# A 32-byte buffer of constants widened to 128 bytes, which moves every on-chip tile behind it by 96 bytes

## The chip, the cores and the metric

The kernel runs on one core of a Trainium2 chip. The metric is device time in microseconds, from one execution of the whole program; the time of a kernel is the median of its runs.

## The reference

Windowed attention with a distance bias, then two feed-forward blocks, all in float32.

```python
batch, n_heads, seq, head_dim = (4, 8, 576, 64)     # q, k, v
scores = scale * np.matmul(q, k.transpose(0, 1, 3, 2))
mask = (rel >= 0) & (rel < 128)
scores = np.where(mask, scores + bias[None], -1000000000.0)
attn = np.exp(scores - max) / (sum + 1e-09)
x = attn @ v                                        # as (2304 tokens, 512)

h = np.maximum(x @ w_in1, 0.0);  x = h * h @ w_out1       # w_in (512, 2048), w_out (2048, 512)
h = x @ w_in2;                   out = (h * np.cos(h)) @ w_out2
```

## The kernel before

**Attention.** The 32 heads are done in 16 pairs. For each pair p TensorE makes the scores of 576 tokens in bands of 192 keys (lines 534 and 543), VectorE adds the bias and takes the row's minimum (line 1089), ScalarE takes the exponent (line 821), GpSimd divides by the row's sum (line 508), TensorE transposes the probabilities (line 589) and multiplies by v (line 631). The probabilities of a pair lie in one of three buffers, probs0 to probs2, taken in turn by p modulo 3. TensorE works on pair s's scores, pair s-2's transposes and pair s-3's values in one turn.

**The two blocks.** They run as 2 x 24 steps (`mlp_step`): three groups of 768 tokens, with eight steps each, per block. A step makes 2 x 128 hidden units. The product with w_in is one level of Strassen's scheme: seven products (`hidden_product`, line 693), each of six matmuls of 384 columns. Float32 is split into a high and a low part in the float32r format, and a product is hi x hi, hi x lo and lo x hi for each of two slices of 128 in the contraction. In the trace's names the moving operand stands first and the weights second: `psum<-xt_hi,comb` streams xt_hi over weights comb.

- The moving high part is always in `xt_hi0` or `xt_hi1` (by the group's parity).
- The moving low part is in `x_lo` for the products 0, 2, 4 and 6 of a step, and in `xt_lo0` or `xt_lo1` for the products 1, 3 and 5.
- The weights are always in `comb`.

After each product stand one to three pieces of the second product (`second_product`). In the first block a piece is three times a 512-column and a 256-column matmul that stream g_hi or g_lo over weights `wout` (lines 732 and 734). In the second block it is the other way round: three 512-column matmuls that stream `wout` over weights g_hi or g_lo (line 727). In a step with `n % STEPS == 1` the pieces stand otherwise: product 0 has three behind it there.

**Where the tiles lie.** `place` hands out addresses within a partition one behind the other, in the order in which it is called, and nothing but the sizes decides them:

```python
            if at is None:
                offset, top[0] = top[0], top[0] + size
```

In the built program `x` starts at byte 16512 = 129 x 128. x, x_lo, raw, sums, angle, the three kept_out tiles, comb, wout and ident lie ahead of `consts`, and all of them start at multiples of 128. `consts` starts at 111232 (also one) and has 32 bytes, of which columns 0 to 2 hold three constants that ScalarE reads as its bias (lines 898, 904, 914). All that is placed behind it starts past a multiple of 32.

The order of work on each of the five engines' queues is written out by hand, and instructions wait on semaphores by count.

Of the kernel before, what the change touches and what calls it, by code (L numbers as in the profile page):

```python
# [15 lines left out]
F32 = mybir.dt.float32  # L16
# [5 lines left out]
P = 128  # L22
# [89 lines left out]
def attention_mlp_kernel(nc, q_t, k_t, v, w_in1, w_out1, w_in2, w_out2, out):  # L112
    with ExitStack() as ctx:
# [3 lines left out]
        def place(name, shape, dtype, at=None):  # L117
            size = 4 * math.prod(shape[1:])
            if at is None:
                offset, top[0] = top[0], top[0] + size  # L120
            else:
                offset, at[0] = at[0], at[0] + size
            return nc.alloc_sbuf_tensor_at(name, shape, dtype, offset=offset)
# [16 lines left out]
        wout = place("wout", [P, W_RING, 2, DM], F32R)  # L140
        wout_raw = place("wout_raw", [P, W_RING, 2, DM], F32, wout_at)
        ident = place("ident", [P, P], F32)
        consts = place("consts", [P, 8], F32)
        part_a = place("part_a", [P, NH], F32)
        part_b = place("part_b", [P, NH], F32)
        xt_hi0 = place("xt_hi0", [P, 7, 2, NH], F32R)
# [1339 lines left out]
```

## Time and profile before

| | |
|---|---|
| runs | 868.67, 868.55, 868.83 us; median 868.67 us |
| profiled execution | 868.67 us, of which its span 866.6 us |
| TensorE busy with matmuls | 852.7 us, 98% of the span |
| weight loads (beside the matmuls) | 768.2 us |
| VectorE, ScalarE, GpSimd busy | 649.2, 525.7, 79.1 us |
| attention alone | about the first 91 us, then overlapped with the first step |

The span runs from the first to the last instruction; the device time is 2.1 us more. "Busy" of TensorE includes the depth of its pipeline: matmuls overlap, so the time that one takes of a stream is read from the start of one to the start of the next, not from its own duration.

### The profile page before, as it was taken

To read this page: it belongs to the slowest core of one execution; us is meant where nothing else is said; L and a number is where in the kernel's file an instruction comes from. 1 tells how busy PE (TensorE), PEld (TensorE's weight loads), DVE (VectorE), ACT (ScalarE), POOL (GpSimd) and SP (SyncE) were. 2 spreads that over 40 slices of the span, in tenths; PEclk is the share of its full clock that TensorE was granted. 3 is DMA by queue.
4 is the path that set the end of the run, shared out by engine and by line. 5 is a ranking of instruction groups with operands and counts; after the bars stand their busy time and mean duration, and the time that the engine had idled before them with its cause. 6 is when DMAs were issued, how large, how long until landed. Compare 5 with 4: busy or idle time off the path is not lost.

```text
span 866.6 us, 16159 instructions
## 1 busy us (share of the span) xinstructions
PE 852.7 (98%) x5844; PEld 768.2 (89%) x5844; DVE 649.2 (75%) x1455; ACT 525.7 (61%) x1145; POOL 79.1 (9%) x174
## 2 busy tenths in 40 slices
PE   7999999999999999999999999999999999999997
PEld 5888998999999999999999989988899898898996
DVE  6999878787677676786776777777877777767664
ACT  7999544342253433343333787777888777777774
POOL 6678600000000000000000000000000000000000
PEclk9999999999999999999999999999999999999999
DMA  6775825647588688688678555555566555664522
GB/s 226 229 250 168 292 84 195 227 166 245 202 291 290 235 305 303 218 290 314 234 254 305 193 181 180 185 196 184 188 236 195 172 178 189 219 230 167 194 73 73
DMA packets 72046, 185.34 MB, mean 214 GB/s; under 512 B 7200, under 2 KB 19488, under 8 KB 69920
## 3 DMA queue, kind: packets, MB, share of 16 engines
q1 hardware_dynamic: 71104, 183.23, 61.8%
q8 instruction: 47, 0.77, 0.4%
q10 hardware_dynamic: 864, 1.08, 0.3%
q14 instruction: 31, 0.25, 0.1%
HBM read 141.82 MB, written 42.47 MB: 213 GB/s over the span
## 4 chain that ended last, share of the span: by engine, by line
PE 89%; DVE 5%; ACT 2%; issue 2%; DMA 1%; DVEq 0%
PE psum L693 37%; PE psum L727 21%; PE psum L732 13%; PE psum L734 7%; PE psum L631 4%; PE psum L589 3%; PE psum L534 3%; DVE hidden_sum L1214 1%; DVE g_lo L1268 1%; DMA wout_raw<-w_out 1%; ACT probs L821 1%; PE psum L543 1%; DVE kept L1193 0%; DVE xt_raw L1133 0%; DMA k_raw<-k_t 0%
## 5 line engine op out<-in xcount | busy, mean ns | idle before, releaser
L693 PE MATMUL psum<-xt_hi,comb 128*128 128x384 f32 x1344 | 397.5, 337 | 3.9 <-DVE hidden_sum L1214 3.7
L693 PEld LDWEIGHTS psum<-xt_hi,comb 128*128 128x128 f32 x1344 | 247.4, 188 | 21.6 <-issue 7.9
L727 PE MATMUL psum<-wout,g_hi 128*128 128x512 f32 x576 | 180.2, 394 | 0.3 <-DVE g_lo L1268 0.3
L732 PE MATMUL psum<-g_hi,wout 128*128 128x512 f32 x384 | 149.8, 393 | 0.0
L1268 DVE TENSOR_TENSOR g_lo<-work,g_hi 128x384 fp32r<-128x384 f32 x192 | 102.5, 553 | 60.2 <-ACT g_hi L922 58.6
L922 ACT ACTIVATE g_hi<-work 128x384 fp32r<-128x384 f32 x192 | 97.0, 516 | 71.4 <-DVE work L1255 39.6
L693 PE MATMUL psum<-x_lo,comb 128*128 128x384 f32 x384 | 129.0, 336 | 0.0
L727 PEld LDWEIGHTS psum<-wout,g_hi 128*128 128x128 f32 x576 | 105.9, 188 | 12.4 <-issue 0.7
L727 PE MATMUL psum<-wout,g_lo 128*128 128x512 f32 x288 | 113.9, 395 | 0.0
L734 PE MATMUL psum<-g_hi,wout 128*128 128x256 f32 x384 | 107.9, 281 | 0.0
L693 PE MATMUL psum<-xt_lo,comb 128*128 128x384 f32 x288 | 96.9, 336 | 0.0
L834 ACT ACTIVATE part_a<-psum 128x384 f32<-128x384 f32 x48 | 23.5, 490 | 100.7 <-PE psum L693 100.6
L732 PEld LDWEIGHTS psum<-g_hi,wout 128*128 128x128 f32 x384 | 71.9, 187 | 9.7
L1214 DVE TENSOR_TENSOR part_b<-psum,part_a 128x384 f32<-128x384 f32 x48 | 26.8, 558 | 65.5 <-PE psum L693 65.5
L693 PEld LDWEIGHTS psum<-x_lo,comb 128*128 128x128 f32 x384 | 72.2, 188 | 3.8
L732 PE MATMUL psum<-g_lo,wout 128*128 128x512 f32 x192 | 75.3, 392 | 0.0
L734 PEld LDWEIGHTS psum<-g_hi,wout 128*128 128x128 f32 x384 | 72.2, 188 | 0.0
L909 ACT ACTIVATE angle<-angle 128x384 f32<-128x384 f32 x96 | 49.8, 519 | 34.9 <-DVE angle L1247 34.7
L508 POOL TENSOR_SCALAR probs<-probs,inverse 128x192 f32<-128x192 f32 (+1 forms) x144 | 67.7, 492 | 20.3 <-DVE inverse L1101 20.3
L727 PEld LDWEIGHTS psum<-wout,g_lo 128*128 128x128 f32 x288 | 54.1, 188 | 12.8
L821 ACT ACTIVATE probs<-probs,neg_max 128x192 f32<-128x192 f32 (+1 forms) x144 | 61.7, 431 | 5.6 <-DVE neg_max L1089 5.6
L914 ACT ACTIVATE angle<-angle,consts 128x384 f32<-128x384 f32 x96 | 59.1, 616 | 2.7
(96 smaller groups left out, 1280.5 us busy)
## 6 DMA issues: line engine op xcount, KB each, us to landing
comb<-comb SPq DMA_DIRECT2D x80, 768.0 KB, 5.0
wout<-wout SPq DMA_DIRECT2D x48, 512.0 KB, 4.9
comb<-comb SPq DMA_DIRECT2D x8, 1792.0 KB, 7.1
comb<-kept SPq DMA_DIRECT2D x8, 1792.0 KB, 6.9
wout_raw<-w_out SPq DMA_DIRECT2D x48, 256.0 KB, 6.2
comb<-comb SPq DMA_DIRECT2D x40, 256.0 KB, 3.1
v_raw<-v SPq DMA_DIRECT2D x16, 512.0 KB, 3.5
raw<-w_in SPq DMA_DIRECT2D x32, 256.0 KB, 7.2
```

The costliest lines, as they stand in the source:

```text
L508: pool.tensor_scalar(m, m, inverse[:, r, u:u + 1], 1.0, ALU.mult, ALU.mult).then_inc(probs_ready, 1)
L631: return pe.matmul(psum[D * h:D * h + D, O_BANK + n % 2, HALF * (n // 2):HALF * (n // 2) + HALF], block, m[block.base_partition():block.ba ...
L693: last = pe.matmul(psum[:, H_BANK + i % 2, 0:NH], wi, mi[:, k, :], start=first, stop=True, skip_group_check=True)
L727: last = pe.matmul(psum[:, Y_BANK + c, :], g[:, r, tok], w, start=start and m == 0, stop=True, skip_group_check=True)
L732: pe.matmul(psum[:, Y_BANK + c, :], wi[:, w], g[:, r, 0:512], start=start and m == 0, stop=True, skip_group_check=True)
L734: last = pe.matmul(psum[:, Y_BANK + 4 + c // 2, 256 * (c % 2):256 * (c % 2) + 256], wi[:, w], g[:, r, 512:N], start=start and m == 0 and c ...
L821: act.activation(m, m, ACT.Exp, bias=neg_max[:, r, u:u + 1], scale=-1.0, accum_out=row_sum[:, r, u:u + 1]).then_inc(exp_ready, 1)
L909: act.activation(a, a, ACT.Abs).then_inc(abs_ready, 1)
L914: act.activation(a, a, ACT.Sin, bias=consts[:, 0:1], scale=-1.0).then_inc(cos_ready, 1)
L922: act.activation(g_hi[:, r, cols], work[i][:], ACT.Copy).then_inc(g_hi_ready, 1)
L1214: dve.tensor_tensor(to, psum[:, H_BANK + bank, 0:NH], left, ALU.add).then_inc(sum_done, 1)
L1268: dve.tensor_tensor(g_lo[:, r, cols], work[i][:], g_hi[:, r, cols].bitcast(F32), ALU.subtract)\
```

## The change

```diff
         ident = place("ident", [P, P], F32)
-        consts = place("consts", [P, 8], F32)
+        consts = place("consts", [P, 32], F32)
         part_a = place("part_a", [P, NH], F32)
```

No instruction is added, removed or moved: the sequence on each of the five engines is the same, shapes and waits too. Only addresses differ, by 96 bytes, for all tiles placed behind `consts`. Where they start in the built programs, as what is left over a multiple of 128 bytes:

| tile | used for | before | after |
|---|---|---|---|
| x, x_lo, comb, wout, ident, raw, sums, angle, kept_out | see above | 0 | 0 (not moved) |
| part_a, part_b, part_c, hidden_sum, work | VectorE, ScalarE | 32 | 0 |
| xt_hi0, xt_hi1, xt_lo0, xt_lo1 | moving operands of line 693 | 32 | 0 |
| g_hi, g_lo | moving (732, 734), weights (727) | 32 | 0 |
| kept | source of a DMA | 32 | 0 |
| probs0, probs1, pt0, pt1, v_raw, v_first | attention | 32 | 0 |
| probs2, q_raw, k_raw, bias, bias_first, bias_tail | attention | 64 | 32 |

The last row is behind `slopes`, which has 32 bytes of its own: the operands of the scores are not at multiples of 128 after the change.

## Rows read from the trace of the kernel before

**Rows 1.** The page's head and its first part: busy time of TensorE.

```profile
span 866.6 us, 16159 instructions
PE 852.7 (98%) x5844; PEld 768.2 (89%) x5844; DVE 649.2 (75%) x1455; ACT 525.7 (61%) x1145; POOL 79.1 (9%) x174
```

**Rows 2.** Windows: busy us (count) of PE, PEld, DVE, ACT, POOL, clock, DMA.

```profile
290.00:490.00 200.00, 199.48 (x1142) 185.19 (x1141) 143.04 (x253) 80.60 (x144) 0.00 (x0) 0.95 0.76 269
520.00:840.00 320.00, 319.48 (x1584) 286.38 (x1583) 234.34 (x452) 245.67 (x464) 0.00 (x0) 0.95 0.56 187
```

**Rows 3.** The waits of PE: us in total, times, longest; its largest.

```profile
PE psum L693 <- DVE hidden_sum L1214: 3.7, 8, 1.1
```

**Rows 4.** Groups by form of PE: busy us, mean ns, idle before.

```profile
L732 PE MATMUL psum<-g_hi,wout 128*128 128x512 f32 x384 | 149.8, 393 | 0.0
L693 PE MATMUL psum<-x_lo,comb 128*128 128x384 f32 x384 | 129.0, 336 | 0.0
L727 PE MATMUL psum<-wout,g_lo 128*128 128x512 f32 x288 | 113.9, 395 | 0.0
L693 PE MATMUL psum<-xt_lo,comb 128*128 128x384 f32 x288 | 96.9, 336 | 0.0
```

**Rows 5.** Timeline of PE in the first block: start, us, what.

```profile
401.57 0.34 PE L693 MATMUL psum<-xt_hi,comb 128*128 128x384 f32 x1
401.75 0.33 PE L693 MATMUL psum<-xt_lo,comb 128*128 128x384 f32 x1
...
402.62 0.39 PE L732 MATMUL psum<-g_hi,wout 128*128 128x512 f32 x1
...
403.66 0.33 PE L693 MATMUL psum<-xt_hi,comb 128*128 128x384 f32 x1
403.83 0.33 PE L693 MATMUL psum<-x_lo,comb 128*128 128x384 f32 x1
...
404.70 0.39 PE L732 MATMUL psum<-g_hi,wout 128*128 128x512 f32 x1
```

**Rows 6.** Timeline of PE in the second block.

```profile
701.93 0.34 PE L693 MATMUL psum<-xt_hi,comb 128*128 128x384 f32 x1
702.12 0.34 PE L693 MATMUL psum<-xt_lo,comb 128*128 128x384 f32 x1
...
703.00 0.62 PE L727 MATMUL psum<-wout,g_hi 128*128 128x512 f32 x2
...
704.39 0.34 PE L693 MATMUL psum<-xt_hi,comb 128*128 128x384 f32 x1
704.57 0.34 PE L693 MATMUL psum<-x_lo,comb 128*128 128x384 f32 x1
...
705.44 0.63 PE L727 MATMUL psum<-wout,g_hi 128*128 128x512 f32 x2
```

**Rows 7.** Timeline of PE in the second block, a step with `n % STEPS == 1`.

```profile
741.45 0.34 PE L693 MATMUL psum<-xt_hi,comb 128*128 128x384 f32 x1
741.62 0.33 PE L693 MATMUL psum<-xt_lo,comb 128*128 128x384 f32 x1
...
742.49 0.62 PE L727 MATMUL psum<-wout,g_hi 128*128 128x512 f32 x2
```

**Rows 8.** Chain that ended last, in the attention: start, us, what.

```profile
64.72 1.04 PE psum L589 x8
...
70.34 1.04 PE psum L589 x8
...
75.96 1.04 PE psum L589 x8
```

**Rows 9.** Groups by form of DVE.

```profile
L1173 DVE TENSOR_TENSOR comb<-raw,comb 128x768 fp32r<-128x768 f32 x8 | 7.6, 953 | 0.0
L1193 DVE TENSOR_TENSOR kept<-raw,kept 128x768 fp32r<-128x768 f32 x8 | 7.6, 952 | 0.0
```

**Rows 10.** DMA issues: count, KB each, median us to landing.

```profile
comb<-comb SPq DMA_DIRECT2D x8, 1792.0 KB, 7.1
comb<-kept SPq DMA_DIRECT2D x8, 1792.0 KB, 6.9
```

## The prediction

> **What bounds the kernel now.** I read the page's first part before anything else, since it tells which engine has no slack: TensorE is busy for 852.7 of 866.6 us [rows 1]. Then the windows, for whether that holds in each stage: in 200 us of the first block it is busy for 199.48, in 320 us of the second for 319.48, while VectorE is busy for 143.04 and 234.34 and ScalarE for 80.60 and 245.67 [rows 2]. So both have over a fifth of each window free. The granted clock is 0.95 of the full 2.4 GHz level in both windows, so the level does not change. Then TensorE's waits: the largest is for VectorE's sums, 3.7 us in all [rows 3]. What decides the time is therefore how fast TensorE streams its operands, and nothing else. That is the one place in which an address could matter, and the rest of the reading is for that.
>
> Own durations are of little use there: they contain the pipeline's depth. I read starts in the timeline. A product of line 693 is six matmuls of 384 columns, and its time is from its first start to the start of what follows it.
>
> - First block: a product with xt_lo runs from 401.57 to 402.62, 1.05 us; the piece behind it, 3 x (512 + 256) columns, to 403.66, 1.04 us; a product with x_lo to 404.70, 1.04 us [rows 5].
> - Second block: a product with xt_lo from 701.93 to 703.00, 1.07 us; two pieces, 6 x 512 columns, to 704.39, 1.39 us; a product with x_lo to 705.44, 1.05 us [rows 6].
> - Second block, another order of pieces: a product with xt_lo from 741.45 to 742.49, 1.04 us [rows 7].
>
> **The change part by part.** No instruction is added or moved, so there is no term for work, and no queue is passed. What is left is the price of a start 32 bytes past a multiple of 128. The trace of before has tiles of both kinds in the same work, so it can be read.
>
> *Moving operands of the hidden products.* In a step 34 of 42 matmuls stream xt_hi or xt_lo, both at 32; the other 8 stream x_lo, at 0. Over 48 steps that is 1632 at 32 and 384 at 0, and the weights, comb, are at 0 for all. A product with x_lo has two matmuls at 0, one with xt_lo has none, and the rest of it is alike. If the start had a price, the products with xt_lo would always be longer by twice that price. They are longer by 0.01 us in the first block and by 0.02 in the second [rows 5, 6], which would make 5 and 10 ns per matmul. But the product with xt_lo at 741.45 takes 1.04 [rows 7], less than the one with x_lo at 704.39, minus 5 ns by the same division. And the same product with xt_lo, with every start the same, takes 1.05, 1.07 and 1.04 us in these three places. Thus where it stands in the sequence moves it by up to 0.03 us, more than the contrast between the tiles. Times are rounded to 0.01 us. The mean durations agree: 336 ns with x_lo and 336 with xt_lo [rows 4]. The two ends of the price are minus 5 and plus 10 ns; I take 0, since the sign changes with the place while the addresses stay.
>
> *The second products.* In the first block g is the moving operand (at 32) and wout the weights (at 0): 2304 columns in 1.04 us are 0.451 ns per column. In the second block wout is the moving operand (at 0) and g the weights (at 32): 3072 columns in 1.39 us are 0.453 ns per column [rows 5, 6]. The durations of 512 columns are 393 and 395 ns [rows 4]. The roles are exchanged and the rate isn't. This does not exclude that both roles cost the same, since one of the two is at 32 in either block; but in the product with x_lo two of six matmuls have both operands at 0, and it takes 1.04 us for 2304 columns, 0.451 ns per column, too. I take 0 for the 1152 matmuls of the first block and the 864 of the second.
>
> *Attention.* The transposes of three pairs in turn, whose probabilities lie in probs buffers at 32, 32 and 64, take 1.04 us for eight each time, and start 5.62 us apart [rows 8]. A weight operand's start at 32 or 64 is worth less than 10 ns in eight. q_raw and k_raw go from 64 to 32, v_raw and pt from 32 to 0; no aligned counterpart exists in the trace for them. Nearest are the hidden products above: 5 ns of 173 is 3%, and of a turn of 5.62 us over 16 pairs that is at most 2.7 us either way. I take 0 for this too, by the transposes.
>
> *VectorE and ScalarE.* The split of the weights takes 953 ns into comb (at 0) and 952 ns into kept (at 32) [rows 9]. Price 0, and it would be covered: VectorE has 57 of 200 us free in the first block [rows 2]. Without that cover, 1 ns on each of its 1455 instructions would be 1.5 us.
>
> *DMA.* Of the moved tiles kept is the large one: eight transfers of 1792 KB out of it take 6.9 us, and the same transfer out of comb, at 0, takes 7.1 [rows 10]. They are covered either way, since TensorE's largest wait is for VectorE [rows 3].
>
> The Trainium skill says otherwise of such a transfer (DMA: Bandwidth & Descriptors, "How a descriptor splits into AXI transactions"): a descriptor that starts off a multiple of 256 bytes fetches from the boundary below it, and the unused bytes cost beats. kept goes from 160 to 0 past such a multiple, so by the page its reads would become a little shorter. The trace has the unaligned one shorter by 0.2 us, so it does not show this; and with TensorE not waiting for it, the sum is the same by either.
>
> The sum: 868.67 + 0. The profiled execution took 868.67 us, 866.6 of span and 2.1 around it, which is also the median of the three runs, so nothing has to be corrected. I say 868.6.
>
> **The rivals.**
>
> *A, faster: the products' time does depend on the placement, in the block where it is longest.* For it: in the second block the products take 1.05 and 1.07, and 1.04 occurs with the same operands [rows 6, 7], so something costs up to 0.03 us there, and the longer ones are those with no moving operand at 0. Against it: the first block has the same starts and does without. If all went at 1.04: 72 products with xt_lo by 0.03 and 96 with x_lo by 0.01 are 2.2 + 1.0 = 3.1 us, to 865.6.
>
> *B, much faster: all that TensorE loses against its clock is the price of the starts.* At 0.95 x 2.4 = 2.28 GHz and one column per cycle six times 384 columns are 1.01 us, 2304 are 1.01 and 3072 are 1.35. Saved: 168 products of the first block by 0.035, 168 of the second by about 0.05, 192 pieces of 2304 columns by 0.03 and 144 times 3072 columns by 0.04, or 5.9 + 8.4 + 5.8 + 5.8 = 26 us, to 843. Against it: matmuls with both operands at 0 do not go faster than the others [rows 5].
> [...]
>
> *C, slower: the pattern of the second block gets into the first.* The place in the sequence decides between 1.04, 1.05 and 1.07, for a reason that the trace doesn't show. If that reason has to do with how the starts of two operands stand to each other, making all equal can put both blocks at the longer values: 72 x 0.02 + 96 x 0.01 = 2.4 us in the first block, to 871.1. It decides from the point where more than 0.005 us is added per product on average (336 x 0.005 = 1.7 us). The operands of the scores, 64 to 32, could add at most 2.7 us in the same direction. Against it: x_lo, comb and wout already start at multiples of 128 together, and their products are among the shortest.
>
> *D: the change doesn't do what it says.* It is so for attention: q_raw and k_raw start at 32 after it. For the blocks the starts do become multiples of 128. D gives 868.7 and can't be told from no effect.
>
> **How the numbers follow.** A measurement here can tell about 0.2% (1.7 us) from no change. No effect, D with it: 0.76, own range 867.1 to 870.3. A: 0.10, B: 0.02, C: 0.12. Half of A stays close enough to be out by more than 0.2% and above 866. So faster by over 0.2% has 0.12, within it 0.76, slower 0.12. The range is 866.0 to 871.0: it holds the first case whole, half of A and most of C, and leaves out B, the rest of A and the far end of C, under 2 in 10.
>
> **What would show it.** In the profile of the changed kernel the products should again be 1.04 to 1.07 us from start to start in the same places as before, 6 x 512 columns 1.39, a turn of the attention 5.62, and the windows 199.5 of 200 and 319.5 of 320. Under A products with xt_lo in the second block fall to 1.04; under B everything, to 1.01; under C products of the first block rise to 1.05 and 1.07. My prediction is wrong if line 693's starts move nearer or farther by more than 1 ns on average with the clock still at 0.95, or if TensorE gets a new wait of over 2 us.

## The result and the profile after

The changed kernel takes 870.79 us (median of 22 runs, 869.26 to 871.35), the kernel before 868.67 us on the same chip. The ratio is 1.0025, with a 95% interval from 1.0018 to 1.0031: slower by 2.1 us, a quarter of a per cent. The forecast was 868.6 us and no effect; 870.79 lies inside the range, but the direction is rival C's.

The page of the changed kernel, head and first part, as [rows 1] of before:

```profile
span 868.9 us, 16159 instructions
PE 853.8 (98%) x5844; PEld 770.1 (89%) x5844; DVE 649.1 (75%) x1455; ACT 525.4 (60%) x1145; POOL 79.3 (9%) x174
```

Nothing is done more often, VectorE and ScalarE are as busy as before, and TensorE still has no slack, as its windows say too (columns as in [rows 2]):

```profile
290.00:490.00 200.00, 199.54 (x1137) 185.35 (x1136) 143.38 (x255) 79.92 (x143) 0.00 (x0) 1.00 0.77 270
520.00:840.00 320.00, 319.57 (x1584) 286.28 (x1583) 234.22 (x453) 245.74 (x465) 0.00 (x0) 1.00 0.57 189
```

What differs in the first window is the count: about five matmuls fewer than in [rows 2] fit into the same 200 us. The granted clock is 1.00 where it was 0.95, and the kernel is slower all the same; more on that below. The timeline of TensorE in the first block, in the places of [rows 5]:

```profile
403.31 0.34 PE L693 MATMUL psum<-xt_hi,comb 128*128 128x384 f32 x1
403.48 0.34 PE L693 MATMUL psum<-xt_lo,comb 128*128 128x384 f32 x1
...
404.36 0.39 PE L732 MATMUL psum<-g_hi,wout 128*128 128x512 f32 x1
...
405.41 0.34 PE L693 MATMUL psum<-xt_hi,comb 128*128 128x384 f32 x1
405.59 0.34 PE L693 MATMUL psum<-x_lo,comb 128*128 128x384 f32 x1
...
406.46 0.40 PE L732 MATMUL psum<-g_hi,wout 128*128 128x512 f32 x1
```

A product is 1.05 us with xt_lo as with x_lo, and the piece between them 1.05. Two decimals are too coarse here. From the starts to the nanosecond, the median over the steps 3 to 23 is 1.039 us before and 1.046 after for a product with x_lo, 1.042 and 1.053 for one with xt_lo. These values are nearly constant: the same from step to step to 1 or 2 ns, outside of the steps with `n % STEPS == 1` and of 13 of the 147 products, which take some 0.08 us more in both kernels. In the second block, in the places of [rows 6]:

```profile
704.20 0.34 PE L693 MATMUL psum<-xt_hi,comb 128*128 128x384 f32 x1
704.37 0.34 PE L693 MATMUL psum<-xt_lo,comb 128*128 128x384 f32 x1
...
705.25 0.62 PE L727 MATMUL psum<-wout,g_hi 128*128 128x512 f32 x2
```

This one is 1.05 us (1.052 in the median) where it was 1.07 (1.062), while the products with x_lo went from 1.049 to 1.054: the second block changed too, but the changes nearly cancel. (Medians of the second block, here and below, are over the steps 26 to 33. With x_lo that before is one of two values: the products 2 and 4 of a step take 1.046 us, 0 and 6 take 1.049.) In the place of [rows 7], the other order of pieces, the product is longer than before, 1.06 for 1.04:

```profile
743.71 0.34 PE L693 MATMUL psum<-xt_hi,comb 128*128 128x384 f32 x1
743.88 0.34 PE L693 MATMUL psum<-xt_lo,comb 128*128 128x384 f32 x1
...
744.77 0.40 PE L727 MATMUL psum<-wout,g_hi 128*128 128x512 f32 x1
```

Where the 2.1 us are is read best from the starts of whole steps, here step 3, step 24 (the first of the second block) and step 46 of the changed kernel:

```profile
138.52 0.41 PE L693 MATMUL psum<-xt_hi,comb 128*128 128x384 f32 x1 [1.18 <-DVE hidden_sum L1214]
...
471.65 0.34 PE L693 MATMUL psum<-xt_hi,comb 128*128 128x384 f32 x1
...
819.48 0.34 PE L693 MATMUL psum<-xt_hi,comb 128*128 128x384 f32 x1
```

and of the kernel before, in the second profile that was taken of it (below):

```profile
138.23 0.41 PE L693 MATMUL psum<-xt_hi,comb 128*128 128x384 f32 x1 [1.12 <-DVE hidden_sum L1214]
...
469.86 0.33 PE L693 MATMUL psum<-xt_hi,comb 128*128 128x384 f32 x1
...
817.34 0.34 PE L693 MATMUL psum<-xt_hi,comb 128*128 128x384 f32 x1
```

A step of the first block went from (469.86 - 138.23) / 21 = 15.792 to (471.65 - 138.52) / 21 = 15.863 us, one of the second from (817.34 - 469.86) / 22 = 15.795 to 15.810. Over 24 steps each that is 1.7 + 0.4 = 2.1 us, the whole loss. Of the longer step of the first block, 66 ns are in its seven hidden products and 6 ns in the pieces between them; in the second block it is 9 and 6 ns. In what follows "step 1" and "step 2" are these two numbers.

### The profile page after: what moved, and what is told of

Its sections match the earlier page's. It is cut to its first block, busy times and chain, and to the rows that moved or that the text cites. A ratio compares the mean times of both kernels' runs of the same rounds, so it can differ in the third digit from the quotient of the medians.

```text
span 868.9 us, 16159 instructions
## 1 busy us (share of the span) xinstructions
PE 853.8 (98%) x5844; PEld 770.1 (89%) x5844; DVE 649.1 (75%) x1455; ACT 525.4 (60%) x1145; POOL 79.3 (9%) x174
## 4 chain that ended last, share of the span: by engine, by line
PE 87%; DVE 7%; issue 2%; ACT 2%; DMA 1%; POOL 0%; DVEq 0%
PE psum L693 37%; PE psum L727 21%; PE psum L732 13%; PE psum L734 7%; PE psum L631 4%; PE psum L589 3%; PE psum L534 2%; DVE hidden_sum L1214 1%; DVE g_lo L1268 1%; DMA wout_raw<-w_out 1%; DVE probs L1089 1%; DVE xt_raw L1133 0%; DVE kept L1193 0%; PE psum L543 0%; DMA k_raw<-k_t 0%
```

## The experiments

### Four other widths of the same buffer

If a start's place over a multiple of 128 bytes were what counts, a shift by 128 would change nothing, and 224 would be as good as 96.

```diff
-        consts = place("consts", [P, 8], F32)
+        consts = place("consts", [P, 16], F32)   # w16; 24, 40 and 64 in w24, w40 and w64
```

> consts is 64 bytes wide, so all that lies behind it is moved by 32 bytes and starts at 64 over a multiple of 128. Theory 1 (the start over a multiple of 128 bytes sets the few ns between matmuls): something between the kernel before and the changed one or of its own, a product of the first block between 1.040 and 1.062 us from start to start, and a turn of the attention between 5.55 and 5.62. Theory 2 (it is the position modulo a longer period or against the tiles that don't move): can't be told apart by this run alone. Rival 3 (the difference is not of the addresses but of how single executions fall out): 868.7, products 1.040 and 1.042 in the first block as before.

> consts is 96 bytes wide, moved by 64 bytes, start at 96 over a multiple of 128. Theory 1: a time of its own, within 2.5 us of the kernel before; the products of the first block a fixed value in all steps. Theory 2: the same. Rival 3: 868.7 and the product times of before.

> consts is 160 bytes wide, moved by 128 bytes: every tile starts at the same place over a multiple of 128 as in the kernel before, but not over a multiple of 256. Theory 1: as before, 868.7 us (within 0.5), products of the first block 1.040 and 1.042 us, a turn of the attention 5.62. Theory 2: differs from before in the product times by 3 ns or more. Rival 3: as before too.

> consts is 256 bytes wide, moved by 224 bytes, all tiles of the blocks start at multiples of 128 as in the changed kernel, but 128 bytes farther. Theory 1: as the changed kernel, 870.8 us (within 0.5), products of the first block 1.046 and 1.053 us, a turn of the attention 5.55. Theory 2: product times of its own. Rival 3: 868.7.

| kernel | shift, bytes | median us | ratio to before (95%) | step 1 | step 2 |
|---|---|---|---|---|---|
| before | 0 | 868.29 | | 15.792 | 15.795 |
| w16 | 32 | 869.51 | 1.0012 (0.9999 to 1.0026) | 15.854 | 15.802 |
| w24 | 64 | 872.75 | 1.0051 (1.0034 to 1.0068) | 15.929 | 15.853 |
| changed kernel | 96 | 870.79 | 1.0025 (1.0018 to 1.0031) | 15.863 | 15.810 |
| w40 | 128 | 867.97 | 1.0003 (0.9994 to 1.0013) | 15.823 | 15.784 |
| w64 | 224 | 866.58 | 0.9978 (0.9966 to 0.9989) | 15.754 | 15.755 |

The changed kernel's own runs of before had 868.67. Theory 1 falls twice. With 224 bytes the blocks' tiles start at multiples of 128 as in the changed kernel, and the time is 4 us less, also less than that of before. And with 128 bytes the total is that of before by accident: a product with x_lo in the first block takes 1.055 us, not 1.039, one with xt_lo in the second 1.046, not 1.062. The effect of a placement is real and of both signs: 6 us lie between w24 and w64. w24 is 4.5 us above before, outside of the 2.5 us that its expectation gave.

### What has a period, and what counts: shifts of 256 and 512, and a shift of everything

```diff
+        consts = place("consts", [P, 72], F32)    # w72: all behind it by 256 bytes; 136 in w136: by 512
```
```diff
+        front = place("front", [P, 24], F32)      # front96: x and all behind it by 96 bytes, consts as before
         x_at = [top[0]]
```

> The kernel before, unchanged, profiled once more. The profile that was shown of it has a granted clock of 0.95 throughout, and a turn of the attention of 5.62 us where four kernels with other addresses have 5.55. If the turn follows the addresses it is 5.62 again; if it belongs to that one execution it is 5.55, with the products of the blocks at 1.039, 1.042, 1.049 and 1.062 us again if these follow the addresses.

> consts is 288 bytes wide, the tiles behind it are moved by 256 bytes. Theory 2a (the period is 256 bytes): product times of the kernel before to 1 ns, and its time within 0.5 us. Theory 2b (the distance to the tiles that don't move matters, without a period of 256): product times of its own. Theory 1 (period 128) was against the run with 128 bytes already and would give those of before here too.

> consts is 544 bytes wide, moved by 512 bytes. If there is a period of 512 bytes: the product times of the kernel before to 1 ns and its time within 0.5 us. If there is none: times of its own, between 864.5 and 873 us as the widths so far.

> consts stays at 32 bytes, and a pad of 96 bytes stands ahead of x, so that every tile, x, comb and wout included, is moved by 96 bytes: the starts of xt and g over a multiple of 128 are those of the changed kernel (0), those of x, comb and wout become 96, and all distances between tiles are those of the kernel before. If distances between tiles that TensorE reads together decide: the product times of the kernel before (1.039, 1.042, 1.049, 1.062) and 868.3 us. If each tile's own start decides: different from both, by 3 ns or more in a product.

| kernel | median us | ratio (95%) | step 1 | step 2 | product times, ns: x_lo, xt_lo; second block x_lo, xt_lo |
|---|---|---|---|---|---|
| before_again | 868.73 (1 run) | | 15.792 | 15.795 | 1039, 1042; 1049, 1062 |
| w72 | 868.06 | 0.9999 (0.9990 to 1.0008) | 15.795 | 15.795 | 1039, 1042; 1049, 1062 |
| w136 | 867.91 | 0.9997 (0.9987 to 1.0007) | 15.791 | 15.795 | 1039, 1042; 1049, 1062 |
| front96 | 867.77 | 1.0000 (0.9990 to 1.0009) | 15.795 | 15.795 | 1039, 1042; 1049, 1062 |

The runs of before beside these three had 868.04 us. All four kernels have the same product times to the nanosecond. The timeline of w72 shows two of them, 401.72 to 402.76 with xt_lo and the next from 403.81:

```profile
401.72 0.34 PE L693 MATMUL psum<-xt_hi,comb 128*128 128x384 f32 x1
401.90 0.33 PE L693 MATMUL psum<-xt_lo,comb 128*128 128x384 f32 x1
...
402.76 0.39 PE L732 MATMUL psum<-g_hi,wout 128*128 128x512 f32 x1
...
403.81 0.33 PE L693 MATMUL psum<-xt_hi,comb 128*128 128x384 f32 x1
```

So at the kernel's own distance the address acts modulo 256 bytes, and it is no single start: in front96 xt and g start at the same place over a multiple of 128 as in the changed kernel, and nothing is lost, because x, comb and wout moved with them. What counts is how the tiles stand to each other. The table of starts modulo 128 hides that: modulo 256, x_lo, comb and wout start at 128 in both kernels, and xt and g go from 160 to 0. I call distance the start of xt or g minus that of comb or wout, modulo 256. It is 32 before (160 against 128), 64 in w16, 96 in w24, 128 in the changed kernel, 160 in w40 and 0 in w64. In the pieces of the second block wout is the moving operand and g the weights, so there the moving operand stands at minus this distance.

before_again was for a second matter. The profile that the prediction was made from has a granted clock of 0.95, here it is 1.00, and the turn of the attention is 5.55 us (60.88 to 66.43 in the chain):

```profile
60.88 2.16 PE psum L631 x64
...
66.43 2.16 PE psum L631 x64
```

It was 5.62 there, and is 5.55 in the median in all 17 other traces of a whole kernel. So the turn belongs to that one execution, and not to addresses, while the product times of the blocks are equal at 0.95 and at 1.00.

### Which tiles

Since 256 bytes are neutral, a group can be moved alone: a pad of 96 bytes ahead of it and one of 160 behind.

```diff
+        place("pad_0", [P, 24], F32); xt_hi0 = place("xt_hi0", [P, 7, 2, NH], F32R)    # xt_only
...
+        place("pad_1", [P, 40], F32); g_hi = place("g_hi", [P, W_RING, N], F32R)
```
```diff
+        place("pad_0", [P, 24], F32); g_hi = place("g_hi", [P, W_RING, N], F32R)       # g_only
...
+        place("pad_1", [P, 40], F32); part_c = place("part_c", [P, NH], F32)
```
```diff
+        place("pad_0", [P, 24], F32); comb = place("comb", [P, 2, 2, 7, 256], F32R)    # comb_only
+        place("pad_1", [P, 40], F32); wout_at = [top[0]]
```
dve_act_only has such pads around part_a and part_b, and around part_c, hidden_sum and work.

> xt_hi and xt_lo (and the tiles of the attention) are moved by 96 bytes, g and all behind it by 256, which left the kernel as it was when all was moved so. Theory 2c (the distance, modulo 256, between the places that TensorE reads at the same time or one behind the other): products of the first block as in the changed kernel, 1.046 and 1.053 us (before 1.039 and 1.042), those of the second 1.052 to 1.054; the second products as before. Time about 870 us, that is most of the loss. Rival: it is the tiles of VectorE and ScalarE (part, hidden_sum, work), then products of before, 868.0.

> g_hi and g_lo alone are moved by 96 bytes, what lies behind them by 256. Theory 2c: the six or three matmuls of a piece take the times of the changed kernel, the products stay near those of before but for the first and last matmul, which stand next to a piece; time within 1.5 us of before. Rival (VectorE's and ScalarE's tiles): as before to the ns.

> comb, the weights of the hidden products, alone is moved by 96 bytes, all behind it by 256. The moving operands keep their distances to one another; only those between moving operands and weights change. Theory 2d (moving against weights): all products change by 3 ns or more in a place, those with x_lo in the matmuls that stream x_lo too. Theory 2e (each moving operand against the one streamed before it): all products to the ns as before, 868.0 us.

> part_a, part_b, part_c, hidden_sum and work alone are moved by 96 bytes, the tiles that TensorE reads by 256. Theory 2c: product times of the kernel before to the ns and 868.0 us. Rival (the tiles of VectorE and ScalarE count): product times and time of the changed kernel, 870.8.

| kernel | median us | ratio (95%) | step 1 | step 2 | product times, ns |
|---|---|---|---|---|---|
| dve_act_only | 868.15 | 0.9996 (0.9985 to 1.0006) | 15.797 | 15.796 | 1039, 1042; 1049, 1062 |
| xt_only | 868.81 | 1.0000 (0.9991 to 1.0010) | 15.874 | 15.750 | 1052, 1056; 1048, 1053 |
| g_only | 868.67 | 0.9995 (0.9986 to 1.0004) | 15.878 | 15.724 | 1050, 1054; 1047, 1045 |
| comb_only | 869.11 | 1.0007 (0.9997 to 1.0017) | 15.821 | 15.809 | 1056, 1039; 1057, 1062 |

The tiles of VectorE and ScalarE do nothing: that rival is out. comb_only leaves the distances between moving operands alone and changes the products, so the moving operand against the weights matters. A product with x_lo of it, 1.06 us for 1.04:

```profile
400.64 0.34 PE L693 MATMUL psum<-xt_hi,comb 128*128 128x384 f32 x1
400.82 0.34 PE L693 MATMUL psum<-x_lo,comb 128*128 128x384 f32 x1
...
401.70 0.40 PE L732 MATMUL psum<-g_hi,wout 128*128 128x512 f32 x1
```

The runs of before beside these four had 868.53 us. My expectation of xt_only missed in the time: it said about 870 us and the second block as in the changed kernel. That of g_only missed too: it said that the hidden products stay near those of before. Their medians went up by 11 and 12 ns in the first block, although none of their own operands moved. The medians hide two values, though. In the steps 3 to 7 a product with xt_lo takes 1.054 or 1.055 us, in the steps 13 to 16 it takes 1.041 or 1.042, the value of before, at the same starts in the same execution. Here is the same product of the steps 5 and 14:

```profile
176.04 0.33 PE L693 MATMUL psum<-xt_hi,comb 128*128 128x384 f32 x1
...
177.09 0.40 PE L732 MATMUL psum<-g_hi,wout 128*128 128x512 f32 x1
...
319.06 0.34 PE L693 MATMUL psum<-xt_hi,comb 128*128 128x384 f32 x1
...
320.10 0.39 PE L732 MATMUL psum<-g_hi,wout 128*128 128x512 f32 x1
```

Outside of the steps with `n % STEPS == 1`, each switch between the two values in the first block (in the steps 8, 11, 12, 19 and 20) stands at one of the long products, of 1.10 to 1.12 us. So the time of a product depends on what is streamed around it as well, and at one placement the stream can run steadily in either of two ways. And no total of the two halves says what both do: xt_only and g_only each have the loss in the first block (15.874, 15.878) and each gain half of it or more back in the second (15.750, 15.724); moved together they take 15.863 and 15.810. The total of each can't be told from that of before, its parts can.

### The other distances, and distance 0 elsewhere

w48 and w56 have 48 and 56 columns of consts. front128_w64:

```diff
+        place("front", [P, 32], F32); x_at = [top[0]]
...
+        consts = place("consts", [P, 64], F32)
```

> consts is 192 bytes wide, moved by 160 bytes; xt and g stand 192 bytes from comb and wout, modulo 256. Theory 2 (distance modulo 256 decides): product times of its own. If the distances act alike on both sides of 0 (192 is 64 short of 256): times like those at 64, 869.5 us; if only 0 is good, between 867.5 and 873.

> consts is 224 bytes wide, moved by 192 bytes; distance 224. If the distances act alike on both sides of 0: as at 32, that is as the kernel before, 868.3 us. Otherwise a time of its own, between 864.5 and 873.

> A pad of 128 bytes ahead of x, and consts 256 bytes wide: all tiles that TensorE reads in the blocks start at multiples of 256 bytes, with distance 0 between them. Theory 2: the product times of the kernel with consts at 256 bytes to the ns (1.041 and 1.041 us in the first block) and its 866.6 us. Rival (the absolute start counts too): another time, 868 or more.

| kernel | distance | median us | ratio (95%) | step 1 | step 2 |
|---|---|---|---|---|---|
| w48 | 192 | 866.20 | 0.9975 (0.9965 to 0.9986) | 15.848 | 15.676 |
| w56 | 224 | 868.54 | 0.9996 (0.9987 to 1.0006) | 15.854 | 15.747 |
| front128_w64 | 0 | 866.79 | 0.9973 (0.9960 to 0.9985) | 15.758 | 15.755 |

The runs of before beside them had 868.83 us. front128_w64 repeats w64 at another absolute start: the same time and the same products, 1.041 and 1.041 us in the first block. w56 has about the total of before at 224, but again by accident, with a longer step 1 and a shorter step 2. The distances are not alike on both sides of 0: 192 is fast and 64 isn't. With 866.20 us w48 is below both times that its expectation gave, 869.5 and 867.5 to 873. w48 and w64 are both faster than before and than the changed kernel, w48 by its second block alone and w64 by both, half each. Of the 0.12 us that a step of w48's second block is shorter, 0.07 are in the pieces. A matmul of 512 columns takes 229.8 ns from start to start in the mean over the steps 26 to 32, and 232.1 before; six of them take 1.38 us, 1.39 in [rows 6]:

```profile
701.49 0.62 PE L727 MATMUL psum<-wout,g_hi 128*128 128x512 f32 x2
...
702.87 0.34 PE L693 MATMUL psum<-xt_hi,comb 128*128 128x384 f32 x1
```

The moving wout stands at -192, that is 64, from g, which is the second-best distance for 512 columns in the bare streams below. w48's median flatters it: seven of its ten runs had a mean granted clock of 0.999 or more and 5 of the 21 of before beside them. Among the runs with such a clock it is 866.0 against 867.5 us, which agrees with the step times ((15.848 - 15.792 + 15.676 - 15.795) x 24 = -1.5 us). For w64 that is 865.1 against 867.5, so w64 is the best placement of the eight. A step of w64's first block, as read from step 3 and step 24, is (469.14 - 138.31) / 21 = 15.754 us:

```profile
138.31 0.41 PE L693 MATMUL psum<-xt_hi,comb 128*128 128x384 f32 x1 [0.89 <-DVE hidden_sum L1214]
...
469.14 0.34 PE L693 MATMUL psum<-xt_hi,comb 128*128 128x384 f32 x1
```

### Bare streams of matmuls

Everything but the matmuls is left out; the kernel fills one moving and one weight tile and stores zeros.

```python
            for ms, ws, n in SECTIONS:            # moving start, weight start, columns
                for i in range(EACH):             # 48 in streams, 32 in streams2
                    m, w = ms[i % len(ms)] // 4, ws[i % len(ws)] // 4
                    pe.matmul(psum[:, i % 2, 0:n], weights[:, w:w + P], moving[:, m:m + n], start=True, stop=True, ...)
```

> This kernel leaves out the whole computation and stores zeros. It streams matmuls of 384 columns, each with its own weight load, 48 for each pair of starts. Theory 2d (moving operand against weights, modulo 256): the interval differs between the distances 0 to 224 by 1 to 8 ns, and is the same where both starts are moved by the same amount (96 and 96, 128 and 128, as 0 and 0; 128 and 96 as 32 and 0). Rival (it takes a change of start from one matmul to the next): all with one pair of starts alike, and longer only in the sections that alternate two starts.

> Leaves out the whole computation and stores zeros. 32 matmuls for each pair of starts, in another order than before. If the distance alone sets the interval: 384 columns at distances 0, 32, 64, 160, 224 at 173.3 to 173.7 ns and at 96 and 128 at 176, whatever stands ahead, and distance 32 at 173.3 for all six weight starts. If what was streamed ahead leaves a state behind: some of the repeated distances differ from the first stream kernel, and the 512-column sections at the same distance differ between their two passes. If the absolute start counts: the six sections at distance 32 differ, and repeat their value where the pair is the same (128 and 96: 176.6).

Each of the two was run once. In the timeline equal matmuls are merged into one row, with the time from the first start to the last end. Four stretches of streams2 with 512 columns, at the distances 192, 0, 64 and 32:

```profile
200.29 6.46 PE L161 MATMUL psum<-moving,weights 128*128 128x512 f32 x27
207.98 6.07 PE L161 MATMUL psum<-moving,weights 128*128 128x512 f32 x26
215.03 6.34 PE L161 MATMUL psum<-moving,weights 128*128 128x512 f32 x27
237.49 6.23 PE L161 MATMUL psum<-moving,weights 128*128 128x512 f32 x26
```

Less one own duration (0.39) and divided by one less than the count, they are 233, 227, 229 and 234 ns from start to start. With all starts, mean ns from start to start after the first four of a section (streams and streams2 where both have it, two passes of the latter for 512 columns):

| distance | 0 | 32 | 64 | 96 | 128 | 160 | 192 | 224 |
|---|---|---|---|---|---|---|---|---|
| 512 columns | 226.9 to 227.6 | 233.3 | 228.9 | 233.7 | 232.4, 233.5 | 234.3 | 233.3 | 233.3 |
| 384 columns | 173.3 to 173.6 | 173.3 or 176.6 | 173.3, 173.4 | 176.6, 176.7 | 175.9 | 173.3 | 174.7 | 173.3, 173.6 |

So one moving operand against one weight operand is enough, and the prices are of the size seen in the kernel: 3 ns of 173, 6 ns of 227. With 96 and 96 or 128 and 128 as the two starts the interval is that of 0 and 0 (173.3, 173.6). For 512 columns the order of the sections made some 1 ns. For 384 columns and distance 32 it isn't so simple. The same two starts, 32 and 0, gave 176.6 behind a section at 96, and 173.3 behind one at 128 and 96:

```profile
113.21 4.58 PE L161 MATMUL psum<-moving,weights 128*128 128x384 f32 x25
...
135.25 4.50 PE L161 MATMUL psum<-moving,weights 128*128 128x384 f32 x25
```

(4.58 - 0.34) / 24 = 177 and (4.50 - 0.34) / 24 = 173 ns. Either value holds for the rest of its section. That the stream ahead picks it is inferred: nothing else in the program differs between the two sections, and in g_only the switches stand at the long products; what exactly picks it is open. At distance 32 from the six weight starts 96, 0, 64, 128, 32 and 160, in this order, three sections had 176.6 and three 173.3 or 173.4, in turn. (The starts 128 and 96 were 176.7 in streams, against its expectation of the 173.3 of 32 and 0.) Neither of the plain theories of streams2's expectation holds: the distance tells most, and at one distance there are two values. Alternating starts could give more than one start, 175.0 for moving starts 0 and 128, 174.4 for weight starts 0 and 32, 176.6 for weight starts 0 and 128, but moving starts 0 and 32 gave 173.3 as one start does.

How far do these intervals carry into the kernel? A product with xt_lo is six matmuls of 384 columns at one distance. Six times the interval of the streams is 1.040 us at 0, 32 (lower value), 64 and 160, 1.048 at 192, 1.055 at 128 and 1.060 at 96. The medians of the first block are 1.041 (w64), 1.042 (before), 1.044 (w16), 1.039 (w40), 1.051 (w48), 1.053 (changed kernel) and 1.058 (w24): all within 4 ns. w56 (224) is the exception with 1.056 for 1.040. And the 1.042 and 1.062 us of before in its two blocks are close to 1.040 and 1.060, the two values of distance 32. The streams don't carry everywhere: with all distances at 0, w64 has products of 1.044 and 1.062 us in its second block (the latter the products 2 and 4 of a step), comb_only has 1.039 with xt_lo at distance 192, and the pieces of w16's first block, with g at 64 from wout, are no shorter than before.

### xt and g at different distances

```diff
+        consts = place("consts", [P, 64], F32)
...
+        place("pad", [P, 48], F32); g_hi = place("g_hi", [P, W_RING, N], F32R)
```

> consts is 256 bytes wide and a pad of 192 bytes stands ahead of g_hi: xt at distance 0 from comb as in the kernel with 256 bytes of consts, g at distance 192 from wout as in the one with 192 bytes. If xt's and g's distances act apart: first block 15.75 to 15.85 us a step, second between 15.64 and 15.74, and 864.5 to 866.5 us in all, no slower than either. If they act together through the sequence: step times outside of these bounds.

The step times are 15.844, inside of the bounds, and 15.758, outside of them: in the first block as w48, which has g's distance, in the second as w64, which has xt's. So the totals are those of the worse half of each, though not made up alike: the pieces of the second block are as much as 52 ns a step shorter than before, and the hidden products, which take 1.044 and 1.063 us by turns there, 15 ns longer. The time is 868.71 us (869.01 for before beside it), ratio 0.9998 (0.9986 to 1.0010), and missed the expectation. The good block of either kernel needs both distances.

## Why the prediction was wrong

- *What bounds the kernel*: right. TensorE's streaming decided, to the last microsecond: 2.1 us in the steps and 2.1 in the result. No wait, no other engine and no DMA took part; the tiles of VectorE and ScalarE alone changed nothing (dve_act_only).
- *Moving operands of the hidden products, "I take 0, since the sign changes with the place while the addresses stay"*: this is the step that failed. It asked what a tile's own start costs, and compared x_lo and xt_lo for that. The runs show no price of a start alone (front96, front128_w64); the distance to the weights has one, and it depends on what is streamed ahead. At constant addresses the product's time already varied between 1.04, 1.05 and 1.07 us; I took this as a reason to call the contrast noise, when nearly constant odd values, the same in step after step, were the effect itself. The size: +7 and +11 ns per product in the first block, more than the 1 ns per start that the prediction names as its sign of being wrong (before_again has before's products at a clock of 1.00, so the clock is not the reason). The bare streams give 2.6 ns for a matmul of 384 columns that goes from distance 32 (at 173.3) to 128 (at 175.9). That is 4 x 2.6 = 10 for a product with x_lo and 6 x 2.6 = 16 with xt_lo: right in sign and order of size, half as much again as measured. If the second block of before runs at the higher value of distance 32 (176.6), the same estimate gives -4 with xt_lo, where -10 was measured: the sign, not the size.
- *The second products, "I take 0"*: the changed kernel's pieces are nearly as before (1.04 and 1.05 us for 2304 columns), since 32 and 128 cost the same for 512 columns (233.3 and 232.4 to 233.5). But the reasoning, exchanged roles and the same rate, compared distance 32 with distance -32, that is 224, both of which are slow. The product with x_lo as a sample of "both at 0" had four matmuls of six at distance 32.
- *Attention*: 0 was right in this sense that the turn is 5.55 us with every placement; the 5.62 of [rows 8] was of that execution alone.
- *VectorE, ScalarE and DMA*: 0 was right. But the prediction reads the two transfers of [rows 10] as an unaligned and an aligned one, in respect of 256 bytes, and they are not: kept starts at 160 past a multiple of 256 and comb at 128. In the changed kernel, where kept starts at 0, its transfers take 6.8 us for 6.9, and 6.8 in before_again too, where it is at 160.
- *Rivals*: C named the mechanism, "how the starts of two operands stand to each other", its place, the first block, and 2.4 us for it; measured are 1.7 there and 0.4 in the second. That the sum is so near is in part luck: C takes all starts to become equal, and by distance they did not, they went from 32 to 128. Where they are equal (w64) the first block is shorter than before. The argument held against C, that x_lo, comb and wout start together and are among the shortest, speaks for a price of distance and not against one. It should have had a larger share than 0.12. A occurred in part in the products with xt_lo of the second block (1.062 to 1.052) and was offset there. B's limit is not reached by any placement: at distance 0 a 512-column matmul still takes 226.9 ns in the streams, 13.6 more than 512 columns at one per cycle of 2.4 GHz (213.3).

## What to carry to other kernels

Where TensorE streams without a gap, the distance modulo 256 bytes between moving operand and weights is a parameter of the kernel, worth some 3% of an interval and here 0.7% between the best and the worst placement; rounding all starts to multiples of 128 is no remedy, as it can give the distance 128. Try equal places modulo 256 first, by padding a small buffer, and then time the eight steps of 32 bytes, since they also act through the order of the stream. Judge an effect of some ns by starts over many steps and by more than one placement, never by a contrast between two tiles in one trace; and look at all the values and not at their median alone, since one placement can have two.

## What was not expected of the hardware

- A stretch of lower clock near the start goes with some 1.5 us more, in some executions of a kernel and not in others. Before: median 867.5 us with a mean granted clock of 0.999 or more (14 runs) and 869.0 below (12 runs), beside w64. Changed kernel: 869.4 (6 runs) and 870.9 (16 runs). The difference between the kernels is 1.9 us in both, so this doesn't explain the result, but a median of few runs can be off by half of the 1.5 us or more. The profiles show where it lies: in the window from 15 to 20 us the clock is 1.00 in w48's and 0.80 in w64's, so that part of the window lay at the 1.2 GHz level in w64's, and TensorE had been busy for 12.12 and 10.49 of the 15 us ahead. Step 3 starts at 137.00 us in w48 and at 138.31 in w64.

```profile
0.00:15.00 15.00, 12.12 (x119) 8.27 (x120) 9.22 (x65) 9.98 (x41) 10.38 (x35) 1.00 0.63 210
15.00:20.00 5.00, 3.24 (x49) 2.48 (x48) 4.06 (x25) 5.00 (x23) 3.52 (x9) 1.00 0.88 286
```
```profile
0.00:15.00 15.00, 10.49 (x120) 6.81 (x120) 9.79 (x71) 10.30 (x43) 10.52 (x36) 1.00 0.67 223
15.00:20.00 5.00, 3.36 (x42) 2.43 (x43) 3.12 (x19) 4.77 (x22) 3.47 (x9) 0.80 0.78 249
```

- In the one execution with a granted clock of 0.95 throughout, the turn of the attention, with its float32 matmuls, was 1.3% longer (5.62 for 5.55 us), and the float32r products of the blocks were not (1.039, 1.042, 1.049 and 1.062 us as at 1.00). Why is open.
- The Trainium skill (TensorE: Matmul & The Clock Gate, "Step-by-step: what each phase is for") says that loading the next weights does not steal read bandwidth from the running matmul, since the two have a read port each. No run here measures bandwidth, but the two reads do not go by unnoticed: the interval follows the distance between their addresses, 226.9 or 233.3 ns for 512 columns. What in the chip does it, and why one placement can have two values, was not found.
